# First expert tile of a chained RWKV, MoE and dense kernel: one half tile gathered from the earlier chunks, the tile worked in halves of 128 and 96 rows

## The reference, cut to what matters

```python
# r, k, v: (4, 8, 768, 48); w, u: (8, 48)
for t in range(768):                                   # per batch and head
    y[t] = r[t] @ (state + (u * k[t])^T v[t])
    state = w * state + k[t]^T v[t]
x = y.transpose(0, 2, 1, 3).reshape(3072, 384)

do = x @ w_skip > 0                                    # mixture of experts, 8 experts
e = argmax(x[do] @ w_gate)
p = softmax(x[do] @ w_gate)[e]
x[do] += p * (relu(x[do] @ w1[e]) @ w2[e])             # w1: 384x1024, w2: 1024x384

h = x @ w_in                                           # 384x2048
out = (h * clip(h + 3, 0, 6) / 6) @ w_out              # 2048x384
```

## Time and profile before

| | us |
|---|---|
| median of 3 runs | 709.5 (709.47 to 711.43) |
| the profiled execution | 706.26 |
| its span in the trace | 704.5 |
| recurrent part on PE, until | 139 |
| list stage, until the first matmul of the first tile | 153 |
| first tile on PE | 152.93 to 170.27 |
| the other tiles, until | 289 |
| dense part, until | 704.5 |

### The profile page before, as it was taken

One profiled execution on the slowest core, in us unless ns is written; L12 is line 12 of the kernel. 1 busy time (PEld: TensorE's weight loads), 2 busy tenths in 40 slices (PEclk: granted clock), 3 DMA queues, 4 the chain that ended last, 5 costly groups with the idle time before them and its releaser, 6 DMA issues.

```text
span 704.5 us, 13935 instructions
## 1 busy us (share of the span) xinstructions
PE 695.5 (99%) x5206; PEld 634.2 (90%) x5206; DVE 383.0 (54%) x802; ACT 322.1 (46%) x704; POOL 138.8 (20%) x190
## 2 busy tenths in 40 slices
PE   7999999999999999999999999999999999999998
PEld 5888888899999999899999999999999989998997
DVE  5677667888888888575443333333333333334332
ACT  4777777725555555554433333333333333323222
POOL 8757876443232221100000000000000000000000
PEclk9999999999999999999999999999999999999999
DMA  7888776627666668300020002000200020001001
GB/s 136 194 208 193 180 171 168 205 87 263 211 223 211 215 212 293 98 1 1 0 90 1 1 0 90 1 0 1 91 1 0 1 91 0 1 1 45 1 1 45
DMA packets 106762, 65.71 MB, mean 93 GB/s; under 512 B 79764, under 2 KB 102296, under 8 KB 106704
## 3 DMA queue, kind: packets, MB, share of 16 engines
q1 hardware_dynamic: 102688, 60.13, 29.9%
q0 software_dynamic: 2560, 4.60, 2.1%
q10 hardware_dynamic: 1456, 0.20, 0.2%
HBM read 53.37 MB, written 12.48 MB: 93 GB/s over the span
## 4 chain that ended last, share of the span: by engine, by line
PE 94%; DVE 3%; issue 1%; POOL 1%; ACT 1%; DMA 0%; DVEq 0%; POOLq 0%; ACTq 0%
PE bank_A L990 8%; PE bank_A L991 8%; PE bank_A L989 8%; PE bank_L L989 4%; PE bank_L L991 4%; PE bank_L L990 4%; PE bank_P L990 4%; PE bank_P L991 4%; PE bank_P L989 4%; PE bank_kT L990 4%; PE bank_kT L991 4%; PE bank_kT L989 4%; PE bank_A L904 3%; PE bank_YT L991 3%; PE bank_YT L990 3%; PE bank_YT L929 3%
## 5 line engine op out<-in xcount | busy, mean ns | idle before, releaser
L1483 DVE TENSOR_TENSOR g_lo<-g,g_hi 128x512 fp32r<-128x512 f32 x96 | 66.5, 692 | 67.0 <-ACT g_hi L774 67.0
L774 ACT ACTIVATE g_hi<-g 128x512 fp32r<-128x512 f32 x96 | 60.7, 632 | 73.1 <-DVE g L1481 73.1
L1481 DVE SCALAR_TENSOR_TENSOR g<-cut,bank_A 128x512 f32<-128x512 f32 x60 | 41.3, 688 | 92.8 <-ACT cut L771 92.8
L771 ACT ACTIVATE cut<-bank_A 128x512 f32<-128x512 f32 x60 | 35.9, 598 | 101.4 <-PE bank_A L991 100.8
L991 PE MATMUL bank_A<-mT_hi,wi_lo 128*128 128x512 f32 x180 | 71.0, 394 | 0.0
L990 PE MATMUL bank_A<-mT_lo,wi_hi 128*128 128x512 f32 x180 | 70.9, 394 | 0.0
L989 PE MATMUL bank_A<-mT_hi,wi_hi 128*128 128x512 f32 x180 | 70.0, 389 | 0.0
L640 ACT ACTIVATE bank_A<-ident,own 128x128 f32<-128x128 f32 x188 | 58.1, 355 | 22.3 <-DVE A_sb L1213 21.7
L1481 DVE SCALAR_TENSOR_TENSOR g<-cut,bank_kT 128x512 f32<-128x512 f32 x36 | 24.8, 688 | 66.6 <-ACT cut L771 66.6
L771 ACT ACTIVATE cut<-bank_kT 128x512 f32<-128x512 f32 x36 | 21.5, 598 | 70.1 <-PE bank_kT L991 70.1
L989 PE MATMUL bank_kT<-mT_hi,wi_hi 128*128 128x512 f32 x108 | 42.1, 389 | 0.9 <-DVE mT_lo L1474 0.9
(11 more groups left out here) (289 smaller groups left out, 1859.0 us busy)
## 6 DMA issues: line engine op xcount, KB each, us to landing
raw<-in_moe_w_dram SPq DMA_DIRECT2D x24, 512.0 KB, 6.4
raw<-in_moe_w_dram SPq DMA_DIRECT2D x7, 1536.0 KB, 6.7
r_in<-in_r_dram SPq DMA_DIRECT2D x24, 192.0 KB, 3.6
v_in<-in_v_dram SPq DMA_DIRECT2D x24, 192.0 KB, 3.5
x_scratch<-y_sb SPq DMA_DIRECT2D x24, 192.0 KB, 2.3
k_in<-in_k_dram SPq DMA_DIRECT2D x23, 192.0 KB, 3.9
m_in<-x_scratch SPq DMA_DIRECT2D x5, 768.0 KB, 5.1
out_dram<-o_sb SPq DMA_DIRECT2D x10, 384.0 KB, 2.7
```

The lines of the kernel that those rows point to most:

```text
L771: eng.activation(cut[f % 2][:, :], p_H[f % 3][:, :], ACT.Relu, bias=0.5, scale=1.0 / 6.0).then_inc(s_cut, 1)
L774: eng.activation(g_hi[f % 4][:, :], g[f % 2][:, :], ACT.Copy).then_inc(s_ghi, 1)
L1481: eng.scalar_tensor_tensor(g[f % 2][:, :], cut[f % 2][:, :], 1.0, p_H[f % 3][:, :], ALU.min, ALU.mult).then_inc(s_g, 1)
L1483: eng.tensor_tensor(g_lo[f % 4][:, :], g[f % 2][:, :], g_hi[f % 4][:, :].bitcast(F32), ALU.subtract).then_inc(s_glo, 1)
```

## The change

**Ranks.** Before the last chunk is routed, DVE works out `skip` = max(0, 1 - n/128), n being the count that the count matmul gives for expert 0 over chunks 0 to 4, a 128th part of what is missing to 128 in each partition. It is added to the running count of expert 0, so that no row of the last chunk gets one of its first 128 ranks. These are two new instructions of DVE and one wait.

**Rows.** The first half tile (128 rows) thus needs neither `in_place` nor the last chunk's rows. POOL gathers it with `listed` itself, as soon as that has landed and the stores of the rows are done but for the last batch's last; the other 96 rows are gathered as before, in front of the last two scatters. `in_place` is 96 wide and `own_slots` has one matmul for a batch in place of two.

**Matmuls.** The first layer of the first tile is worked for the 128 rows and for the 96 rows apart, 72 matmuls each, with four of the eight hidden pieces side by side in one bank. The high by high and high by low products of the first half stand ahead of the second half's transposes. The second layer has its three kinds of products one after the other, and not piece by piece. `ON` is (8,).

**Splits.** The high parts of w2 are made by ACT early, the hidden values are evicted in four instructions (four pieces at once), and DVE does the low parts of the first rows and of w1 ahead of the plan. `last_w`, `last_id` and `goes_to`, made in every tile before, are made in the last tile alone.

The diff below has the filler, then GpSimd, ScalarE, TensorE and VectorE.

```diff
-ON = (40, 9, 5)
+ON = (8,)
+            eng.wait_ge(s_tok, N_TOK + 4)
             eng.wait_ge(s_listed, 16)
+            for b in range(B):
+                eng.wait_ge(s_st[b], 16 * (NC - b // (B - 1)))
+            rows_of(0, 0, listed, stored=N - P)
             scatters(NC - 1, NC - 1, range(0, LATE))
-            eng.wait_ge(s_tok, N_TOK + 4)
             for b in range(B):
                 eng.wait_ge(s_st[b], 16 * NC)
             eng.wait_ge(s_who0, 1)
-            fetch(0)
+            rows_of(0, 1, who[0])
             scatters(NC, NC - 1, range(LATE, B))
             n_tiles = tiles_planned(eng)
...
-            incoming(0, 0, 0)
+            rows_high(0, 0)
+            eng.wait_ge(s_raw2, 16 * W2_PARTS)
+            for f in range(G1 - 2):
+                w2_high(f)
+            rows_high(0, 1)
+            for f in range(G1 - 2, G1):
+                w2_high(f)
+            for t in range(TH):
+                for part in range(2):
+                    eng.wait_ge(s_h0, 2 * t + part + 1)
+                    eng.activation(hT_hi[:, part * FB:(part + 1) * FB, t * P:t * P + TW[t]],
+                                   p_h0[t][part][:, 0:FB * TW[t]].rearrange("p (f t) -> p f t", f=FB), ACT.Relu).then_inc(s_hhi0, 1)
             n_tiles = tiles_planned(eng)
...
-            rows_T(0, 0, 0, first=True)
-            go_on(ON[TH], p_YT)
-            first_tile()
+            half_T(0, 0, 0)
+            go_on(ON[0], p_kT)
+            eng.wait_ge(s_rows, NT)
+            eng.wait_ge(s_gTlo, 1)
+            first_half(0, w1_hi, xgT_hi)
+            first_half(0, w1_hi, xgT_lo)
+            half_T(0, 0, 1)
+            first_half(0, w1_lo, xgT_hi)
+            eng.wait_ge(s_who0, 2)
+            eng.wait_ge(s_rt, routed(NC + 1, 1))
+            eng.wait_ge(s_gTlo, TH)
+            first_half(1, w1_hi, xgT_hi)
+            first_half(1, w1_hi, xgT_lo)
+            first_half(1, w1_lo, xgT_hi)
             n_tiles = tiles_planned(eng)
...
+            def first_half(t, w1_part, x_part):
+
+                for f in range(G1):
+                    for kc in range(KC):
+                        if w1_part is w1_lo:
+                            eng.wait_ge(s_w1lo, kc + 1)
+                        a = eng.matmul(p_h0[t][f // FB][:, f % FB * TW[t]:(f % FB + 1) * TW[t]], w1_part[:, kc, f * P:(f + 1) * P],
+                                       x_part[:, kc, t * P:t * P + TW[t]], start=w1_part is w1_hi and x_part is xgT_hi and f % FB == 0 and kc == 0,
+                                       stop=w1_part is w1_lo and kc == KC - 1, skip_group_check=True)
+                    if w1_part is w1_lo and f % FB == FB - 1:
+                        a.then_inc(s_h0, 1)
+                return a
...
+                    eng.tensor_scalar(skip[:, :], p_count[:, B, 0:1], -1.0 / P, 1.0, ALU.mult, ALU.add).then_inc(s_skip, 1)
                     carry(c)
+                    eng.wait_ge(s_skip, 1)
+                    eng.scalar_tensor_tensor(choice[:, 0, 0:1], skip[:, :], 0.0, choice[:, 0, 0:1], ALU.max, ALU.add).then_inc(s_skip, 1)
+                    eng.wait_ge(s_skip, 2)
...
-                        eng.tensor_scalar(in_place[b][:, :], token[:, 0:TT], place[:, b:b + 1], None, ALU.is_equal).then_inc(s_in_place, 1)
+                        eng.tensor_scalar(in_place[b][:, :], token[:, P:TT], place[:, b:b + 1], None, ALU.is_equal).then_inc(s_in_place, 1)
...
             eng.wait_ge(s_listed, 16)
-            eng.tensor_copy(listed_f[:, :], listed[:, :, 0]).then_inc(s_listed_f, 1)
+            eng.tensor_copy(who[0][:, 0, :], listed[:, 0, :])
+            eng.tensor_copy(listed_f[:, :], listed[:, 1, 0:1]).then_inc(s_listed_f, 1)
```

More of the change, by code:

```diff
@@ L38 @@
 EC = NK * TH
+assert NK * TT >= N + P and TH == 2
 BASE = NK * TT // P
@@ L196, in chained_moe_program @@
         assert (NK + MAXT) * E <= BLK
-        in_place = [nc.alloc_sbuf_tensor_at(f"in_place{b}", [P, TT], F32, offset=at_hi + b * TT * 4) for b in range(B)]
+        in_place = [nc.alloc_sbuf_tensor_at(f"in_place{b}", [P, TT - P], F32, offset=at_hi + b * TT * 4) for b in range(B)]
         at_lo = nc.sbuf_base
@@ L965, in own_slots @@
                 eng.wait_ge(s_in_place, b + 1 + b // LATE + 1)
-                for t in range(TH):
-                    m = eng.matmul(p_own[0:TW[t], t, :], in_place[b][:, t * P:t * P + TW[t]], own_rows[:, b, :], start=b == 0 and t == 0,
-                                   stop=b == B - 1, skip_group_check=True)
-                return m
+                return eng.matmul(p_own[0:TW[1], :], in_place[b][:, :], own_rows[:, b, :], start=b == 0,
+                                  stop=b == B - 1, skip_group_check=True)
             def go_on(times, where):
@@ L1023, in first_layer @@
                 for f in range(G1):
-                    wait(eng, s_hlo, G1 * j + (f - 1 if f < 2 else f - 2))
+                    wait(eng, s_hlo, G1 * (j - 1) + (f - 1 if f < 2 else f - 2))
                     for kc in range(KC):
@@ L1051, in second_layer @@
                     wait(eng, s_y2ev, TH * j + t + 1 - TH)
[L1052 removed]
+                    if of_first:
+                        first_second(t, hT_hi, w2_hi)
+                        first_second(t, hT_lo, w2_hi)
+                        a = first_second(t, hT_hi, w2_lo)
+                    for f in () if of_first else range(G1):
                         if t == 0:
[L1054 removed]
+                            eng.wait_ge(s_hlo, G1 * (j - 1) + f + 1)
                             eng.wait_ge(s_w2lo, G1 * j + f + 1)
@@ L1392, in incoming @@
                     rows_low(j, t)
+            rows_low(0, 0)
+            split_w1(0, range(1, KC))
             shape3 = [P, MAXT, E]
```

123 lines of the change are left out of this document (68 added, 55 removed).

## The result

The changed kernel takes 715.1 us as a median (714.05 to 715.74), the kernel before 709.47 us beside it (709.28 to 711.43). The ratio is 1.0071, with a 95% interval from 1.0054 to 1.0088. The forecast was 712.3 us with a range up to 714.0: the sign was right, the size was not, and the time lies above the range. The two profiled executions are further apart than the medians: 714.21 us with a span of 712.4 against 706.26 with 704.5, so the spans differ by 7.9 us. Both differences have to be explained.

The account below looks back on a forecast made before the run. TensorE bounds the kernel, about 7.5 us of its idle time hidden by filler. Starting 5.2 us earlier against 8.0 us more matmuls gives +2.8: 709.1 us profiled, 712.3 us as a median, range 709.0 to 714.0.

Parts of the forecast that it names:

- Start of the first half: First tile: gather issued at 142.62 us, rows there at 146.0, first matmul at 147.7.
- rival of late rows: First tile: gather starts no earlier than before, sum starts at 151.9, +7.0 us, 716.5; chance 0.09 together with late weights.
- Price of a matmul: First layer, first tile: the weight load sets 0.1115 us for each of 144 matmuls, whatever moves.
- 9-column stream: Earlier plain fp32 matmuls with 9 moving and 128 stationary columns: 0.111 us each, taken to show that loads bind.
- moving-columns rival: First layer's halves: moving columns set the price, 0.063 and 0.049 us a matmul, median 706.8 us; chance 0.10.
- the one between: First layer's halves: loads partly overlap, break-even 0.092 us a matmul, no difference, 708.7 at 0.087 us; chance 0.06.
- Second layer and second tile: First tile's second layer starts at 164.1 us and takes 8.97; the second tile starts at 173.05.
- the sum: First tile up to the second tile's start: 5.2 us earlier start, 8.0 us more matmuls, +2.8 us.
- The late plan: DVE's plan ends at 155.9, 6 us later; SP served by 158.0 at the latest, PE not held at second tile.
- the second half, 72 x 0.1115 = 8.03: First tile's first layer for the other 96 rows: 8.03 us of matmuls, ending at 164.1.
- the baseline: Whole kernel: median 3.2 us above the profiled 706.26 us; the same 2.8 us added to the median, giving 712.3.

Follow-up runs that it names:

- padded kernel: The changed kernel with the second half's 72 matmuls moving 128 columns in place of 96, the extra left out at eviction; 709.46 us, ratio 1.0051 to the kernel before.
- mixed order: The changed kernel with 384-column matmuls of the first half's second layer between the second half's 96-column products; 711.98 us, ratio 1.002, repeated at 711.45 us, 1.0021.
- two tuned versions: The changed kernel with one 224-column first-layer pass, second rows' low part earlier, filler 28 and 9 (ratio 0.9979) or 20 and 7 (0.9949, repeated 0.996).

## Why the prediction was right and wrong

**Start of the first half: right where DVE doesn't stop and the clock doesn't fall in the list stage.** 148.06 and 148.04 against 147.7, and the gather is issued at 142.84 against 142.62 even with the stop. On a chip with the stop the first half starts at 149.3 to 149.6 (149.55 in the first result), a small case of the rival of late rows, by another cause than it named. Where the clock fell ahead of it, it came as late as 148.84 on a quiet chip and 150.13 on the other kind.

**Price of a matmul: right.** The 9-column stream was the row that decided. The run that widened the moving part to 224 and the one that narrowed it to 64 change the price by 0.001 us (0.110 and 0.112 against 0.111), which refutes the moving-columns rival and the one between. The latter had its break-even at 0.092 us, and nothing came near. The forecast also named the Trainium skill's sustained figure for 128 columns, about 81 ns ("TensorE: Matmul & The Clock Gate", section "Back-to-back issue gap"). The measurement, 111 ns with fp32r operands, lies above it.

**Second layer and second tile: right without the clock.** The padded kernel has them 0.3 and 0.4 us behind the forecast. It costs 709.46 - 706.0 = 3.5 us where the sum had 2.8, and its second tile is 173.48 - 170.27 = 3.2 later; 0.35 of the excess is the start's.

**The late plan: right.** SP fetched the second tile's first weights at 159.32 us where I had 158.0 at the latest; that is 1.3 later, less than the 1.85 by which the whole tile started later, and PE never waited for them. Only the mixed order, whose PE is earlier there, waits 0.2 us for the low rows.

**First failed step: the sum took the full clock for granted.** It costed "the second half, 72 x 0.1115 = 8.03" and no rival named the clock. They took 168.00 - 157.86 = 10.1 us in the first result, and the second layer behind them was slowed too. The row of 96-column matmuls drops the clock, every time: in all five traces with 72 matmuls of 96 or 64 columns in a row (the changed kernel three times, with more filler, with 64 columns), in the row's second or third product. Half clock lasts 6.8 to 13.7 us, into the second layer. From the start of the first half to the second tile this costs, against the padded kernel, 3.2 us in the first result (3.3 by the rows above), 4.8 in both repeats and with 64 columns, and 6.4 with more filler. All 21 executions of these kernels have a mean clock of 0.995 or less. In none of the two traces with 128 columns there, the one with 224, or the two with 384-column matmuls in between does the clock fall in the tile, and of their 38 executions 35 have 0.997 or more. What the runs show is that the fall goes with a long row of narrow moving parts behind full weight loads, while PE shows no gap. The Trainium skill ("TensorE: Matmul & The Clock Gate", sections "What's actually happening" and "HAM oscillation — how this bites in real kernels") says that the gate looks at how busy PE has been, and gives idle gaps as what closes it. Here filling the gaps didn't help and widening the moving part did, so a PE that the profile calls 100% busy isn't safe. Which quantity the chip takes as busy no run here tells, nor whether the type or the other engines have a part in it.

**Second failed step: the baseline.** "The median of the three runs lies 3.2 us above it, and I add the same 2.8" treated the 3.2 as an offset of every kernel. It isn't. Where DVE stops for 2.3 to 2.6 us, the kernel before loses 710.2 - 706.0 = 4.2 us or, with 709.5, 3.5. The one trace of it there has its gather 149.97 - 146.77 = 3.2 us later, of which some 0.4 are the half clock in the list's last matmuls, 1.44 us for 1.00. Its executions at full clock, at 709.35 us, lose 3.3. So about 3 us go with the stop, and the rest of the median's loss with the executions whose clock falls. That the stop is all of the 3 is argued, not shown. The changed kernel gathers by `listed` and loses only the 1.2 to 1.5 us by which its first half starts later (149.3 to 149.6 against 148.06), and its time hardly differs, 715.1 and 715.5 against 714.6. That is why the same change costs 8.6 us on one chip (ratio 1.0126) and 5.6 on others (1.0071 and 1.008). On a quiet chip the changed kernel's second tile is 178.27 - 173.05 = 5.2 us behind the forecast, 4.8 of it the clock and 0.4 the start. On a chip with the stop part of this is given back, since the baseline stands higher. The size was wrong by 2.8 us only because one missing term was partly paid by the other.

**What stays open.** What the stop of DVE and PE at 140.2 us is: it ends at the same time in both kernels, its releaser is none that the profile knows, and it is absent on the two quiet chips. Why the clock of before falls there in 17 of 45 executions and in none on the quiet chips is open too.

## What to carry to other kernels

Cutting a tile along its moving side repeats every weight load. The second part alone then costs as much as the whole (164.39 - 156.35 = 8.04 us for 128 columns, and 8.03 for 224), so starting early with the first part gains nothing unless that part ends before the whole could have begun. Gather early, but multiply in one pass: the two tuned versions of that are 0.2 to 0.5% faster than the kernel before, on three chips, though part of this may be their smaller filler. Untuned it won nothing.

Where narrow matmuls with full weight loads can't be avoided, mix wide ones into the row, or pad the narrow ones if the load binds anyway; mixing took the loss from 0.8 to 0.2% on one chip, padding from 1.3 to 0.5% on another.

If the profiled execution lies well off the median of the same kernel, the trace may lack something that most runs have, as here DVE's stop. A term for it belongs into the range, and not the same for both kernels.

## What was not expected of the hardware

- More work was faster: with 96 columns moved in the second pass the ratio on a quiet chip is 1.0126, with 128 or 224 it is 1.0051, and PE is busy all along in each from the first half to the second tile.
- A matmul of 128 stationary columns takes 0.110 to 0.112 us with 64, 96, 128 or 224 moving columns at full clock, and 0.213 at half, measured with 64 and 96.
- Filler of 128-column transposes doesn't always keep the clock: in four traces it fell in the list stage or at the first rows, between 145.7 and 147.6 us, after a wait of PE of 0.8 to 1.4 us (others had such a wait and no fall), and in one of these 40 transposes took 7.38 us instead of 4.57. Filler counted in instructions stretches with the clock, and can end after what it was to bridge.
- A stop of 2.3 to 2.6 us on DVE, ending at 140.0 to 140.3 us, in every trace on some chips and in none on others. PE has one of 0.4 to 0.7 us that ends then too, in all of these traces but that of the mixed order's repeat, where PE ran at half clock at that time.
